# Splitting w_in and w_out2 ahead of the second MLP of an attention and two-MLP kernel: more parts on GpSimd, high parts outside the gates

## The reference, cut to what matters

```python
def reference(...):                        # all arrays float32
    attn_out = _attn_ref(q, k, v, proj)    # (2, 8, 768, 64), masked by hash buckets
    x = attn_out.transpose(0, 2, 1, 3).reshape(1536, 512)
    # first MLP, d_ff 768
    h = np.maximum(np.maximum(x @ w1, x @ w2), x @ w3)
    y = h @ moe_w_out
    # second MLP, d_ff 2048
    h = y @ moe2_w_in
    g = h * (1.0 / (1.0 + np.exp(-1.702 * h)))
    return g @ moe2_w_out
```

## Time and profile before

| | us |
|---|---|
| median of 3 runs (lowest, highest) | 691.15 (690.58, 692.47) |
| the profiled execution | 690.5 |
| its span, first to last instruction | 688.7 |
| busy in the span: PE / DVE / GpSimd / ACT | 669.2 / 483.1 / 469.2 / 343.6 |
| mean granted TensorE clock, share of full speed | 0.993 |

### The profile page before, as it was taken

One profiled execution on the slowest core, in us unless ns is written; L12 is line 12 of the kernel. 1 busy time (PEld: TensorE's weight loads), 2 busy tenths in 40 slices (PEclk: granted clock), 3 DMA queues, 4 the chain that ended last, 5 costly groups with the idle time before them and its releaser, 6 DMA issues.

```text
span 688.7 us, 11930 instructions
## 1 busy us (share of the span) xinstructions
PE 669.2 (97%) x3874; PEld 579.6 (84%) x3874; DVE 483.1 (70%) x971; ACT 343.6 (50%) x755; POOL 469.2 (68%) x539
## 2 busy tenths in 40 slices
PE   7899999999999999999999999789999999999998
PEld 5777776867777799999999999679988888988986
DVE  5777787788788799879698763555666666545454
ACT  3777877777777630010104353545554465544433
POOL 4766756688885899878852356887677776877610
PEclk9999999999999999999999999899999999999999
DMA  4836737548243111111110200132222215222102
GB/s 110 196 87 140 170 89 169 133 112 184 68 113 116 32 30 32 31 32 32 46 46 2 93 1 30 63 95 89 61 61 62 61 31 185 62 67 74 45 1 91
DMA packets 58700, 54.12 MB, mean 79 GB/s; under 512 B 28944, under 2 KB 47632, under 8 KB 58640
## 3 DMA queue, kind: packets, MB, share of 16 engines
q1 hardware_dynamic: 58320, 53.36, 28.6%
q10 hardware_dynamic: 320, 0.01, 0.0%
HBM read 32.51 MB, written 3.15 MB: 52 GB/s over the span
## 4 chain that ended last, share of the span: by engine, by line
PE 81%; POOL 8%; DVE 5%; ACT 2%; issue 2%; DMA 1%; SPq 0%; ACTq 0%; DVEq 0%; POOLq 0%
PE psS L1324 9%; PE psO L1346 9%; PE psR L1332 9%; PE psR L1392 6%; PE psR L1393 6%; PE psR L1394 6%; PE psS L1392 6%; PE psS L1393 6%; PE psS L1394 6%; POOL w_lo L678 3%; PE psS L1493 3%; PE psS L1492 3%; PE psS L1491 3%; POOL w_parts L683 2%; PE psR L1293 2%
## 5 line engine op out<-in xcount | busy, mean ns | idle before, releaser
L549 POOL TENSOR_SCALAR probs<-probs,lone,inv 128x768 f32<-128x768 f32 x96 | 94.0, 987 | 60.9 <-DVE inv L1009 60.9
L678 POOL TENSOR_TENSOR w_lo<-w_raw,w_hi 128x256 fp32r<-128x256 f32 x96 | 78.4, 824 | 35.9 <-ACT w_hi L877 35.2
L991 DVE TENSOR_REDUCE neg_max<-psS 128x1 f32<-128x768 f32 x96 | 91.1, 950 | 13.1 <-PE psS L1324 9.9
L734 ACT ACTIVATE probs<-psS,neg_max 128x768 f32<-128x768 f32 x96 | 86.5, 901 | 21.7 <-DVE neg_max L991 21.7
L524 POOL TENSOR_SCALAR w_hi<-w_raw 128x256 fp32r<-128x256 f32 (+1 forms) x79 | 48.7, 620 | 53.5 <-PE psS L1394 32.2
L1332 PE MATMUL psR<-ident,probs 128*128 128x128 f32 x576 | 74.7, 273 | 2.2 <-ACT w_raw L727 0.9
L743 ACT ACTIVATE probs_t<-psR 128x384 f32<-128x384 f32 x128 | 59.5, 491 | 31.1 <-PE psR L1332 31.1
L1332 PEld LDWEIGHTS psR<-ident,probs 128*128 128x128 f32 x576 | 66.6, 140 | 6.8 <-POOL probs L549 3.7
L1346 PE MATMUL psO<-probs_t,v_raw 128*64 128x384 f32 x384 | 68.8, 494 | 0.0
L1208 DVE TENSOR_TENSOR v_raw<-psR,early 128x384 f32<-128x384 f32 x64 | 35.5, 554 | 38.3 <-PE psR L1394 37.8
L877 ACT ACTIVATE w_hi<-w_raw 128x256 fp32r<-128x256 f32 x87 | 34.1, 408 | 50.3 <-POOL w_raw L669 32.0
(11 more groups left out here) (258 smaller groups left out, 1881.6 us busy)
## 6 DMA issues: line engine op xcount, KB each, us to landing
w_raw<-in_moe_w_in SPq DMA_DIRECT2D x16, 512.0 KB, 3.5
w_raw<-in_moe_w_out SPq DMA_DIRECT2D x32, 256.0 KB, 2.7
w_raw<-in_moe_w SPq DMA_DIRECT2D x9, 512.0 KB, 3.8
h_lo<-w_hi SPq DMA_DIRECT2D x22, 192.0 KB, 3.4
h_hi<-w_hi SPq DMA_DIRECT2D x18, 192.0 KB, 3.4
w_raw<-in_q SPq DMA_DIRECT2D x16, 192.0 KB, 3.3
w_raw<-in_k SPq DMA_DIRECT2D x16, 192.0 KB, 4.1
v_raw<-in_v SPq DMA_DIRECT2D x16, 192.0 KB, 2.6
```

The costliest lines, as they stand in the source:

```text
L549: pool.tensor_scalar(probs[i % PROBS][:, :], probs[i % PROBS][:, :], lone[:, i % 6:i % 6 + 1], inv[:, i % 6:i % 6 + 1], ALU.add, ALU.mult) ...
L678: pool.tensor_tensor(in2_slot(w_lo, n, which), in2_raw(n, PARTS2[which]), f32(in2_slot(w_hi, n, which)), ALU.subtract).then_inc(in2_split, 1)
L734: act.activation(probs[i % PROBS][:, :].rearrange("p (a b) -> p a b", a=2), psS[i % 2][:, :, 0:HALF], ACT.Exp, bias=neg_max[:, i % 6:i % 6 ...
L991: dve.tensor_reduce(neg_max[:, i % 6:i % 6 + 1], psS[i % 2][:, :, 0:HALF], AX.XY, ALU.min).then_inc(max_ready, 1)
```

## The change

GpSimd makes the high part of all fourteen parts of blocks 0 and 1 (POOL_PARTS 11 becomes 14). Its list takes w_out2's low chunks 0 and 1 behind part (1,1), ahead of parts (1,2) to (1,6). From block 2 on its order stays. On ACT, w_out2's high chunks 0 and 1 go into the w_out stage, behind first_copy(0); in2_hi(1,4) to (1,6) fall away; in2_hi of parts 1 to 4 of block n+1 stand together in period n behind g_hi(n-1,3), and none is left among the sigmoids. The sums of y for the second half go one to a period: the sums on DVE in periods 1 to 4 behind mix(n,0), the high parts on ACT in periods 2 to 5, the low parts on DVE in periods 3 to 6 behind mix(n,1).

```diff
--- before.py
+++ after.py
@@ -69,7 +69,7 @@
 
     FIRST_MIX = {2 * OUTS * B - 4: (0,), 2 * OUTS * B - 3: (1, 2), 2 * OUTS * B - 2: (3, 4), 2 * OUTS * B - 1: (5, 6)}
 
-    POOL_PARTS = 7 + 4
+    POOL_PARTS = 2 * 7
     T_ORDER = [(0, 1), (0, 2), (0, 3), (0, 4), (1, 1), (1, 3), (1, 2), (1, 4)]
     RING = 3
     MARKS = 2 * 6
@@ -683,28 +683,35 @@
                 pool.tensor_tensor(w2_parts[:, g % W2_SLOTS, 1, :], out2_raw(g), f32(w2_parts[:, g % W2_SLOTS, 0, :]),
                                    ALU.subtract).then_inc(out2_split, 1)
 
-            def in2_first_parts(n):
+            def in2_first_sums(n):
                 pool.wait_ge(in2_loaded[n % 2], 16 * (n // 2 + 1))
                 in2_sum(n, "s1", "a21", "a22", ALU.add)
                 in2_lo(n, 0)
                 in2_sum(n, "s3", "a11", "a21", ALU.subtract)
                 pool.wait_ge(in2_summed, 4 * n + 1)
                 in2_sum(n, "s2", "s1", "a11", ALU.subtract)
-                for which in range(1, 4):
-                    in2_lo(n, which)
 
             def in2_last_sum(n):
-                in2_lo(n, 4)
                 pool.wait_ge(in2_summed, 4 * n + 3)
                 in2_sum(n, "s4", "a12", "s2", ALU.subtract)
 
-            in2_first_parts(0)
-            in2_last_sum(0)
-            in2_lo(0, 5)
-            in2_lo(0, 6)
-            in2_first_parts(1)
-            for n in range(MIXES):
+
+            for n in range(2):
+                in2_first_sums(n)
+                in2_lo(n, 1)
+                if n == 1:
+                    out2_lo(0)
+                    out2_lo(1)
+                for which in range(2, 5):
+                    in2_lo(n, which)
+                in2_last_sum(n)
+                in2_lo(n, 5)
+                in2_lo(n, 6)
+            in2_first_sums(2)
+            for n in range(1, MIXES):
                 if n + 1 < MIXES:
+                    for which in range(1, 5):
+                        in2_lo(n + 1, which)
                     in2_last_sum(n + 1)
                 out2_lo(2 * n)
                 out2_lo(2 * n + 1)
@@ -712,7 +719,7 @@
                     in2_lo(n + 1, 5)
                     in2_lo(n + 1, 6)
                 if n + 2 < MIXES:
-                    in2_first_parts(n + 2)
+                    in2_first_sums(n + 2)
 
 
         @block.scalar
@@ -930,42 +937,36 @@
                         y_sum_hi(0, t)
                 if n == 2 * OUTS * B - 4:
                     first_copy(0)
+                    out2_hi(0)
+                    out2_hi(1)
             g_hi(0, 0)
             sigmoid(0, 1)
             g_hi(0, 1)
-            in2_hi(1, 4)
-            out2_hi(0)
-            out2_hi(1)
             sigmoid(0, 2)
             g_hi(0, 2)
-            in2_hi(1, 5)
-            in2_hi(1, 6)
 
             for n in range(1, MIXES):
                 sigmoid(n - 1, 3)
-                if 1 < n < MIXES - 1:
-                    in2_hi(n + 1, 4)
                 first_copy(n)
                 g_hi(n - 1, 3)
-                if n == 1:
-                    for which in range(5):
-                        in2_hi(2, which)
                 if n == FPS2 + 1:
                     copy_result(0, COPIES[0][2])
+                if n == 1:
+                    in2_hi(2, 0)
+                if n + 1 < MIXES:
+                    for which in range(1, 5):
+                        in2_hi(n + 1, which)
                 out2_hi(2 * n)
                 out2_hi(2 * n + 1)
                 if n + 1 < MIXES:
                     in2_hi(n + 1, 5)
                     in2_hi(n + 1, 6)
-                if n in (4, 5):
-                    for t in T_ORDER2[2 * n - 8:2 * n - 6]:
-                        y_sum_hi(1, t)
+                if 2 <= n < 6:
+                    y_sum_hi(1, T_ORDER2[n - 2])
                 if n + 2 < MIXES:
                     in2_hi(n + 2, 0)
                 for which in range(3):
                     sigmoid(n, which)
-                    if n + 2 < MIXES:
-                        in2_hi(n + 2, which + 1)
                     g_hi(n, which)
                 if n == FPS2:
                     copy_result(0, COPIES[0][0])
@@ -1252,8 +1253,14 @@
                 g_lo(n - 1, 3)
                 if n == FPS2 + 1:
                     copy_result(0, COPIES[1][2])
-                for which in range(4):
-                    mix(n, which)
+                mix(n, 0)
+                if n < 5:
+                    y_sum(1, n - 1)
+                mix(n, 1)
+                if 3 <= n < 7:
+                    y_sum_lo(1, n - 3)
+                mix(n, 2)
+                mix(n, 3)
                 gate(n, 0)
                 mix(n, 4)
                 g_lo(n, 0)
@@ -1263,12 +1270,6 @@
                 gate(n, 2)
                 mix(n, 6)
                 g_lo(n, 2)
-                if n in (3, 4):
-                    y_sum(1, 2 * n - 6)
-                    y_sum(1, 2 * n - 5)
-                elif n in (5, 6):
-                    y_sum_lo(1, 2 * n - 10)
-                    y_sum_lo(1, 2 * n - 9)
                 if n == FPS2:
                     copy_result(0, COPIES[1][0])
             gate(MIXES - 1, 3)
```

## The result

The changed kernel takes **683.79 us** (median of five runs, 683.02 to 685.37), the kernel before 690.58 in the five runs beside them (689.47 to 692.47). The ratio is 0.9904, with a 95% interval of 0.9881 to 0.9927: faster by 6.8 us. 681.5 was forecast, from a median before of 691.15, with a range from 679.9 to 685.3. The run that was profiled took 683.02, with a span of 681.2. GpSimd's lines are where they were.

What follows compares the result with a forecast made beforehand. PE bounds the kernel; only its stalls and slow clock could be won, 9.99 us. Terms -3.95, -2.0, -2.06, -1.16, -0.84, +0.4 sum to -9.6: 690.5 becomes 680.9, the median 0.65 above, 681.5 us; range 679.9 to 685.3.

Steps and rivals of the forecast that it cites:

- out2(0,0)'s stop: PE's 3.78 us idle ahead of the first out2(0,0), with a matmul's tail, would go: -3.95 us.
- The slow clock: Some four microseconds at 1.2 GHz after PE's 3.78 us stop, ten matmuls, would go: about -2.0 us.
- The 1.63 us ahead of up2(1,0): PE's idle there, from mix(0,5) behind gate(0,1), would stay; it could shrink by 0.5 us, no more.
- The high parts, -2.06, -1.16, -0.84: With ACT's high parts out of the gates, waits at periods 2, 7 and 8 go: -2.06, -1.16, -0.84 us.
- the label: "POOL w_lo" on three later PE stops, disbelieved; as rival, PE does wait for GpSimd's low parts: 686.7 us, chance 0.06.
- The added wait in steady periods: ACT's wait for sum s4 now precedes sigmoid(n,0), which stays PE-bound with 0.5 to 1.3 us over: no cost.
- The slower rival: ACT's wait for s4 ahead of sigmoid(n,0) decides every period, taking 5.0 us more: 692 us and more, chance 0.04.
- Period 1, +0.4 (0 to 0.8): In period 1 sigmoid(1,0) starts at +11.9 to +13.0 against +12.2: +0.4 us, between 0 and 0.8.
- Six steps of 0.55: Sigmoid, gate, mix(n,4), sigmoid, gate, mix(n,5) ahead of PE's next period: some 0.55 us each, 3.3 in all.
- The bound of 3.8: Period 1's stall if four gate steps and one y sum held GpSimd their whole length: 3.8 us, giving 684.9.
- y's sums, "nothing": Sums of y one a period, and their low parts, fall where DVE waits for products: no cost.
- gates still late in part: Another ACT or DVE wait: periods 6, 7 keep their 2.0, or period 1 loses 3.4 more; 683.5 to 684.9, chance 0.12.

Runs made afterwards that it cites:

- the run with this part alone: Kernel before, with only w_out2's first parts moved: out2_hi(0), (1) behind first_copy(0), out2_lo(0), (1) behind part (1,1): 690.01 us, ratio 0.9986.
- the repetition: The changed kernel, unaltered, run again beside a later variant on one chip: 685.14 us (683.14 to 685.88, six runs).
- s4 late: Changed kernel, in period 1 alone ACT's in2_hi(2,5), in2_hi(2,6), in2_hi(3,0) moved from ahead of sigmoid(1,0) to behind g_hi(1,1): 682.70 us, ratio 0.9880.
- the high parts alone: Kernel before, with only ACT's in2_hi of parts 1 to 4 moved together behind g_hi(n-1,3), from block 3 on: 687.48 us, ratio 0.9948.
- GpSimd held: Changed kernel, with GpSimd in period 1 starting the sums of block 3 only after gate(1,2): 683.69 us, ratio 0.9895.
- ACT copies: Changed kernel, with POOL_PARTS back at 11 and ACT making high parts (1,4), (1,5), (1,6) in its idle places: 684.21 us, ratio 0.9897.
- y's sums alone: Kernel before, with only the y sums of the second half put one to a period: 689.49 us, ratio 0.9980.

## Why the prediction was right or wrong

1. **out2(0,0)'s stop, -3.95: right**, also in its reason, a matter of order on GpSimd. out2_lo(0) and (1) ran at 422.49 for 2.55 us into idle time of GpSimd, of which 2.01 us were still left until 427.05. But the run with this part alone shows that the term was not a term by itself: the later stop takes it back unless the high parts move too. The sum had both, so nothing was lost by it.
2. **The slow clock, -2.0: right in the profiled execution** (1.00 through period 1), and in the repetition. It is not safe: two variants had 0.50 behind stops as long as the new one of 1.95 us. The clock goes with the spread of the changed kernel's runs: of its eleven, the two with a mean granted clock of 1.000 are the fastest (683.02 and 683.14), and the nine with 0.995 to 0.998 took 683.38 to 685.88. Only two of the eleven have a profile, so where the others lost their clock stays open.
3. **The 1.63 us ahead of up2(1,0): as said**, 1.63 again.
4. **The high parts, -2.06, -1.16, -0.84: right**, with the label distrusted for the right reason. Two runs bear that out: moving ACT's queue alone (s4 late) shortened a stop with this label, and the high parts alone removed three of them.
5. **The added wait in steady periods: right.** Periods 6 and 7, and all from 8 on, take 15.68 or 15.69 us. The slower rival needed 5 us more per period, and nothing of it came.
6. **Period 1, +0.4 (0 to 0.8): here the prediction failed.** It was +3.14, and +0.33 more in period 2 and +0.17 in period 5. By the forecast's own steps, sigmoid(1,0) was to start at +11.9 to +13.0 and had to start by +12.2; it started at +13.64. Six steps of 0.55 were to take 3.3 us; they took 5.04. The start was 1.4 us too late and the steps 1.74 us too long: together the 3.14. The start was also 0.6 past the top of its own range. For the start, GpSimd's list from part (1,2) on (427.05) to the end of s4 (443.24) took 16.2 us, where 14.5 to 15.6 had been worked out (427.91 to 442.4 or 443.5). The late part lies at its beginning, where 4.64 us had been given to the work ahead of (1,5), and 5.26 passed (427.05 to 432.31). There too GpSimd met DVE:

```profile
429.62 0.70 POOL L524 TENSOR_SCALAR w_hi<-w_raw 128x256 fp32r<-128x256 f32 x1
...
431.10 1.05 POOL L669 TENSOR_TENSOR w_raw<-w_raw 128x256 f32<-128x256 f32 x1
```

The copy takes 0.41 elsewhere and the sum 0.74. The meeting with y's sum, 0.7, was inside the range. For the steps, the forecast took "the 8.9 us that I moved already hold such meetings" as a reason to price none on DVE. That was the wrong side: GpSimd's length held them, DVE's did not. Counted from start to start, the first gate took 0.7 us more than its 0.55 and the second 0.5 more. Another 0.5 is a step that the list of six does not have: ahead of gate(1,1) stands g_lo(1,0) on DVE, and it ended at 447.87, when sigmoid(1,1) had been done since 447.20. With the high parts among the gates, as it was, the mean gate took 658 ns; the change moves just these. The bound of 3.8 in the same paragraph was the better number.
7. **y's sums, "nothing": wrong in detail.** They cost 0.7 in period 1 and, put into the kernel before, removed two stops that the forecast had given to the high parts alone.

So of the 9.6 us forecast, 3.24 didn't come (2.74 in period 1, 0.5 in periods 2 and 5). The profiled executions still differ by 7.5, not by 6.4. Up to 1.1 of that belongs to no step of the change: up2(1,0) starts 0.86 us earlier after (430.67 against 431.53), and the difference is there ahead of all that was edited (an h_hi copy of ACT at 412.43 against 413.29; the first moved instruction follows at 413.86). So it is by luck that the profiled run came within 2.1 us of its forecast (683.0 against 680.9), where the steps missed 3.24. One thing that goes with it is seen in the trace, a slow stretch near the program's start, in the kernel before and not in the changed one:

```profile
16.00:24.00 8.00, 7.46 (x37) 6.44 (x38) 5.64 (x16) 5.19 (x12) 3.38 (x4) 0.79 0.63 157
```

```profile
16.00:24.00 8.00, 6.67 (x41) 5.26 (x40) 6.38 (x16) 5.65 (x13) 4.30 (x4) 1.00 0.64 160
```

The repetition of the changed kernel has a slow stretch there too (0.91 and 0.93 up to 20 us), so it comes and goes with the execution. Where mix(0,5) kept its place, up2(1,0) started at 430.63 to 431.54 in the six profiles with 1.00 in the first 24 us, and at 431.53 to 432.47 in the four with a slow stretch. The clock isn't all: with GpSimd held it started at 431.46, at a clock of 1.00. What else differs there stays open. Of the rivals, "gates still late in part" (683.5 to 684.9) named what came: its first form, the periods 6 and 7, didn't happen, its second, period 1 with 3.4 us more, came at 2.74 more. The Trainium skill (SBUF — State Buffer, "SBUF: two separate sides") was quoted for 684.9 by its lock rule. This case agrees with the rule in direction: DVE's 0.55 and GpSimd's 0.74 became 1.09 and 1.06 where they met. In period 1 the two gates and the g_lo took 0.54 to 0.77 longer each, about the length of one 256-column operation of GpSimd (0.74); two of the six steps, the mixes, which read PSUM, stayed at 0.54.

## What to carry to other kernels

A wait that is removed is worth its length only if the next engine's work is there in time: list, for the stage behind it, when every in-order queue reaches its next wait, and put ahead of each critical instruction nothing that waits for an engine running late. When an engine's waits are moved, price what it will now run beside: an operation that was cheap because its neighbour began behind it doesn't stay cheap when the neighbour is already under way. And distrust a releaser that ended at the same moment as another candidate; moving one queue's instructions tells the two apart.

## What was not expected of the hardware

- **How far DVE and GpSimd lengthen one another.** A gate of two SBUF inputs took 0.55 alone, 1.09 beside 256-column operations of GpSimd, 1.32 across the end of a 512-column one and the start of the next, 1.64 beside the 512-column ones; GpSimd's sum took 1.06 instead of 0.74 beside a g_lo and a gate, and 1.46 beside y's sum. A mix, which reads PSUM, took 0.54 to 0.56 throughout. Over the whole tail the mean gate went from 658 to 782 ns, with the number of gates the same; what differs is how many of them began with a GpSimd operation under way, 15 or 37.
- **The clock after a stop of about 1.9 us** was 1.00 in the kernel before (1.89), in the changed one (1.95) and in its repetition, and fell to 0.50 in the run with GpSimd held (1.93) and in the run with ACT copies (1.92). With y's sums alone it was 1.00 after a stop of 2.48. The length of the stop alone doesn't decide it; what does stays open.
- **The first 24 us** hold a slow stretch in some executions and not in others, whatever the kernel (0.79 from 16 to 24 us before, 1.00 after). Between the two it goes with 0.86 us in the start of up2(1,0), as much as the term for period 8, and it belongs to no edit.
